# Strassen's scheme for two MLPs over pairs of batches, and attention in head pairs

## What is computed

```python
q_n, k_n = rmsnorm(q, g_q), rmsnorm(k, g_k)          # q, k, v: (4, 12, 448, 64)
attn = softmax(q_n @ k_n.T / 8);  x = attn @ v       # then x: (4, 448, 768)
xn = (x - mean) / sqrt(var + 1e-6) * g_ln            # first MLP
x = x + relu(xn @ w_ch1) @ w_ch2                     # 768 -> 3072 -> 768
u = x + (x.T @ U @ V).T                              # mixing over the 448 rows, rank 32
out = u + relu(u @ w2_ch1) @ w2_ch2                  # second MLP
```

## Time and profile before

| | us |
|---|---|
| runs before, median of 3 | 1796.21 (1795.0 to 1798.2) |
| profiled execution, span | 1794.6 |
| TensorE busy | 1766.4 |
| VectorE busy | 913.4 |
| ScalarE busy | 706.3 |
| GpSimd busy | 202.1 |

### The profile page before, as it was taken

The page is one execution under the profiler, slowest core; times in us unless marked ns, Lnnn a source line. Parts: engine busy times, 40 slices in busy tenths (PEclk is TensorE's granted clock), DMA queues, the critical chain, the costliest instruction groups (busy, mean ns, idle before and its releaser), DMA issues.

```text
span 1794.6 us, 29017 instructions
## 1 busy us (share of the span) xinstructions
PE 1766.4 (98%) x10272; PEld 1655.9 (92%) x10272; DVE 913.4 (51%) x1595; ACT 706.3 (39%) x1268; POOL 202.1 (11%) x201
## 2 busy tenths in 40 slices
PE   6999999999999999999999999999999999999998
PEld 5999999899999999999999999999999999999997
DVE  7999999743344444444444444444433433343332
ACT  5777777522333323332333233323222322232221
POOL 6666666000000000000000000000000000000000
PEclk9999999999999999999999999999999999999999
DMA  2222224233333233333333333332433333333320
GB/s 73 69 69 72 68 71 139 87 106 116 113 106 103 93 111 101 106 106 106 105 108 100 102 100 106 106 106 89 138 121 106 97 131 121 106 99 128 121 88 31
DMA packets 205744, 180.41 MB, mean 101 GB/s; under 512 B 12497, under 2 KB 179281, under 8 KB 205649
## 3 DMA queue, kind: packets, MB, share of 16 engines
q1 hardware_dynamic: 203280, 173.51, 30.3%
q10 hardware_dynamic: 2368, 5.51, 0.8%
HBM read 173.48 MB, written 5.51 MB: 100 GB/s over the span
## 4 chain that ended last, share of the span: by engine, by line
PE 80%; DVE 0%; issue 0%; ACT 0%
PE h_ps L733 39%; PE y_ps L750 38%; PE h_ps L680 1%; PE h_ps L669 1%; PE h_ps L698 1%; PE h_ps L706 0%; PE y_ps L658 0%; DVE in_nat L891 0%; ACT in_hi L786 0%; DVE in_lo L854 0%; DVE in_lo L851 0%; DVE y_t L927 0%
## 5 line engine op out<-in xcount | busy, mean ns | idle before, releaser
L844 DVE TENSOR_TENSOR w_lo<-w_raw,w_hi 128x768 fp32r<-128x768 f32 x190 | 182.0, 958 | 674.0 <-ACT w_hi L782 674.0
L750 PE MATMUL y_ps<-h_hi,w_hi 128*128 128x448 f32 x1152 | 424.4, 368 | 0.0
L733 PE MATMUL h_ps<-in_hi,w_hi 128*128 128x448 f32 x1152 | 415.9, 361 | 3.1 <-DVE in_lo L851 1.1
L733 PE MATMUL h_ps<-in_hi,w_lo 128*128 128x448 f32 x1152 | 417.9, 363 | 0.0
L750 PE MATMUL y_ps<-h_hi,w_lo 128*128 128x448 f32 x1152 | 417.8, 363 | 0.0
L750 PE MATMUL y_ps<-h_lo,w_hi 128*128 128x448 f32 x1152 | 417.7, 363 | 0.0
L733 PE MATMUL h_ps<-in_lo,w_hi 128*128 128x448 f32 x1152 | 417.4, 362 | 0.0
L781 ACT ACTIVATE w_hi<-w_raw 128x768 fp32r<-128x768 f32 x189 | 159.7, 845 | 538.1 <-PE y_ps L750 538.1
L817 ACT ACTIVATE h_hi<-h_ps 128x448 fp32r<-128x448 f32 x192 | 104.7, 545 | 380.1 <-PE h_ps L733 338.5
L733 PEld LDWEIGHTS h_ps<-in_hi,w_hi 128*128 128x128 f32 x1152 | 215.6, 187 | 19.1 <-DVE in_lo L851 1.5
L733 PEld LDWEIGHTS h_ps<-in_lo,w_hi 128*128 128x128 f32 x1152 | 216.2, 188 | 15.8
(11 more groups left out here) (90 smaller groups left out, 1407.3 us busy)
## 6 DMA issues: line engine op xcount, KB each, us to landing
w_raw<-in_moe_w_ch SPq DMA_DIRECT2D x384, 384.0 KB, 3.8
qk_raw<-in_q SPq DMA_DIRECT2D x48, 112.0 KB, 2.0
qk_raw<-in_k SPq DMA_DIRECT2D x48, 112.0 KB, 2.1
qt_raw<-in_q_t SPq DMA_DIRECT2D x48, 112.0 KB, 2.5
v_nat<-in_v SPq DMA_DIRECT2D x48, 112.0 KB, 2.0
out<-o_nat ACTq DMA_DIRECT2D x12, 336.0 KB, 5.0
out<-in_nat ACTq DMA_DIRECT2D x4, 336.0 KB, 3.1
u_sb<-in_moe_U SPq DMA_DIRECT2D x4, 56.0 KB, 2.5
```

Of the source, the lines that this page charges most:

```text
L733: last = nc.tensor.matmul(h_ps[j % 2][:, :S], w[:, j % NW, c, :], x[:, c, :], start=(c == 0 and t == 0), stop=(c == DC - 1 and t == 2))
L750: last = nc.tensor.matmul(y_ps[c][:, :S], w[:, j % NW, c * P:(c + 1) * P], x[:, j % 2, :], start=(j == 0 and t == 0), stop=(j == FC - 1 an ...
L844: nc.vector.tensor_tensor(w1_lo[:, r], w1_raw[:, r], w1_hi[:, r].bitcast(F32), ALU.subtract)
```

## The change

Both parts are written anew.

**MLPs.** Four units (`s` = 0 to 3) take two batches through one MLP each. Each product of 2x2 blocks is made with seven block products (P1 to P7) for eight, by Strassen's scheme in Winograd's form. The left factor is the weights, the right one the activations; both need sums of blocks first, and the seven products are combined after. An up-group ("G", 12 in a unit) has 3 blocks of depth, 9 matmuls a product; a down-group ("M", 18 in a unit) has 2 blocks of depth, 6 matmuls. The list `prods` sets one order for all engines: two up-groups, the first two products of the next, three down-groups. Six PSUM banks go round; P2, P3 and P4 are added onto the bank of P1, P5 and P7 after these were read (`ONTO`). The sums of weights (`weight_sum`) and of the hidden values (`hidden_sums`) are made on GpSimd, as are the low parts of P4's weights, the last of each group (`ON_POOL`); the other low parts (`weight_low`, L1063) on VectorE, 384 columns for G and 256 for M. `combine` and `gather` read the products on VectorE. The input of the next unit is split (`make_high`, `make_low`) beside the last 21 products. Results stand transposed in SBUF (`acc`) and go through DRAM (`xres`, `xnrm`) between units. The mixing has 12 items of two blocks, spread over the units 1 and 2.

**Attention.** 24 pairs of heads, 96 steps of 2 x 112 rows. The scores are six matmuls of 448 columns with 64 rows each (`score`, L705), head 0 in rows 0 to 63 and head 1 in 64 to 127. One maximum (L1003) covers both heads. The low part of q is made on GpSimd, and the power there is over 16 columns. x is turned back and normalised here (L736), not in the MLPs. Inputs arrive in other layouts, and the output leaves transposed.

```diff
+P1, P7, P6, P5, P2, P3, P4 = range(7)
+ORDER = {"G": (P1, P7, P6, P5, P2, P3, P4), "M": (P1, P5, P6, P2, P7, P3, P4)}
+ONTO = {P2: P1, P3: P5, P4: P7}
+LAST_IN_BANK = (P6, P2, P3, P4)
+HEAD = 2
+ON_POOL = {("G", P4), ("M", P4)}
...
+    for s in range(STAGES):
+        for j in range(NJ):
+            for g in (2 * j, 2 * j + 1):
+                prods += [("G", s, g, k) for k in ORDER["G"][HEAD if g == 2 * j and j else 0:]]
+            if j + 1 < NJ:
+                prods += [("G", s, 2 * j + 2, k) for k in ORDER["G"][:HEAD]]
+            prods += [("M", s, j * NM + m, k) for m in range(NM) for k in ORDER["M"]]
+    number = {p: q for q, p in enumerate(prods)}
...
+    for s in range(1, STAGES):
+        first = number["M", s - 1, NJ * NM - NM, P1]
+        anchors = (first + 3, first + 8, first + 12)
...
+                def squares(t):
...
+                    raw = qk[:, t % 2].rearrange("p a h i d -> p (a h i d)")
+                    nc.gpsimd.tensor_tensor(qk_sq[:].rearrange("p a h i d -> p (a h i d)"), raw, raw,
+                                            ALU.mult).then_inc(sq_done, 1)
...
+                def weight_sum(r, k):
...
+                    if k == P5:
+                        out, in0, in1, op = s1, a21, a22, ALU.add
+                    if k == P7:
+                        out, in0, in1, op = a21, a11, a21, ALU.subtract
...
+                    if k == P6:
+                        out, in0, in1, op = s2, s1, a11, ALU.subtract
...
+                    if k == P3:
+                        out, in0, in1, op = weights(product_of(r, P3)), a12, s2, ALU.subtract
...
+                    nc.gpsimd.tensor_tensor(out, in0, in1, op).then_inc(sum_done, 1)
+                def weight_low(q):
+                    pool.wait_ge(whi_done, q + 1)
+                    w = width(q)
+                    nc.gpsimd.tensor_tensor(w_lo[:, q % RING, :w], weights(q), w_hi[:, q % RING, :w].bitcast(F32),
+                                            ALU.subtract).then_inc(wplo_done, 1)
+                def hidden_sums(q):
+                    if (g := group_past(q, 1)) is not None:
+                        pool.wait_ge(relu_done, 4 * g + 3)
+                        if g:
+                            pool.wait_ge(hlo_done, cut(g - 1, P5))
+                        nc.gpsimd.tensor_tensor(t_t1, t_c12, t_b11, ALU.subtract).then_inc(th_done, 1)
+                        pool.wait_ge(th_done, 4 * g + 1)
+                        nc.gpsimd.tensor_tensor(t_c12, t_c22, t_t1, ALU.subtract).then_inc(th_done, 1)
+                        pool.wait_ge(th_done, 4 * g + 2)
+                        pool.wait_ge(hlo_done, cut(g, P1))
+                        nc.gpsimd.tensor_tensor(t_b11, t_c12, t_b11, ALU.subtract).then_inc(th_done, 1)
+                    if (g := group_past(q, 3)) is not None:
+                        pool.wait_ge(th_done, 4 * g + 3)
+                        pool.wait_ge(relu_done, 4 * g + 4)
+                        pool.wait_ge(hlo_done, cut(g, P2))
+                        nc.gpsimd.tensor_tensor(t_c21, t_c21, t_c12, ALU.subtract).then_inc(th_done, 1)
...
-                    lhs = q_st[:, slot, i * TP:(i + 1) * TP]
-                    nc.tensor.matmul(scores[i][:TP, :S], lhs, k_hi[:, slot, :], start=True, stop=False)
-                    nc.tensor.matmul(scores[i][:TP, :S], lhs, k_lo[:, slot, :], start=False,
-                                     stop=True).then_inc(scores_done, 1)
+                def score(n):
...
+                    for a, b in ((q_hi, k_hi), (q_hi, k_lo), (q_lo, k_hi)):
+                        for h in range(2):
+                            rows = slice(h * D, (h + 1) * D)
+                            last = nc.tensor.matmul(mm_ps[:TP, 2 * (n % 2) + h, :S], a[rows, t % 2, i * TP:(i + 1) * TP],
+                                                    b[rows, t % 2], start=a is q_hi and b is k_hi, stop=a is q_lo)
+                    last.then_inc(s_done, 1)
...
-                terms = ((w1_hi, in_hi), (w1_hi, in_lo), (w1_lo, in_hi))
...
-                    for t, (w, x) in enumerate(terms):
-                        last = nc.tensor.matmul(h_ps[j % 2][:, :S], w[:, j % NW, c, :], x[:, c, :],
-                                                start=(c == 0 and t == 0), stop=(c == DC - 1 and t == 2))
-                    for t, (w, x) in enumerate(terms):
-                        last = nc.tensor.matmul(y_ps[c][:, :S], w[:, j % NW, c * P:(c + 1) * P], x[:, j % 2, :],
-                                                start=(j == 0 and t == 0), stop=(j == FC - 1 and t == 2))
+                def product(q):
+                    kind, s, n, k = prods[q]
+                    weights_split(pe, q)
+                    if before[q] is not None:
+                        read_out(pe, before[q])
...
+                    for c in range(chunks):
+                        if kind == "G" and n == 0:
+                            pe.wait_ge(inlo_done[c], made(s, k))
+                        for p, (w, x) in enumerate(((w_hi, x_hi), (w_hi, x_lo), (w_lo, x_hi))):
+                            last = nc.tensor.matmul(bank(q), w[:, q % RING, c * P:(c + 1) * P], x[:, k, c],
+                                                    start=k not in ONTO and c == 0 and p == 0,
+                                                    stop=c == chunks - 1 and p == 2, skip_group_check=k in ONTO)
+                    last.then_inc(prod_done, 1)
...
+                    nc.vector.reduce_max(nmax[:, n % 2], mm_ps[:TP, 2 * (n % 2):2 * (n % 2) + 2, :S], axis=AX,
+                                         negate=True).then_inc(max_done, 1)
...
+                def weight_low(q):
+                    dve.wait_ge(whi_done, q + 1)
+                    w = width(q)
+                    nc.vector.tensor_tensor(w_lo[:, q % RING, :w], weights(q), w_hi[:, q % RING, :w].bitcast(F32),
+                                            ALU.subtract).then_inc(wlo_done, 1)
...
+                    nc.vector.tensor_tensor(in_lo[:, k, c], src, in_hi[:, k, c].bitcast(F32),
+                                            ALU.subtract).then_inc(inlo_done[c], 1)
+                    nc.vector.tensor_tensor(h_lo[:, k, g % 2], src, h_hi[:, k, g % 2].bitcast(F32), ALU.subtract
+                                            ).then_inc(hlo_done, 1)
+                def combine(q):
+                    g, k = g_no(q), prods[q][3]
...
+                    dve.wait_ge(prod_done, q + 1)
+                    if k == P6:
+                        dve.wait_ge(p1_done, g + 1)
+                        nc.vector.tensor_tensor(t_u2, bank(q), t_u2, ALU.add).then_inc(comb_done, 1)
+                        dve.wait_ge(comb_done, 5 * g + 1)
+                        wait(dve, th_done, 4 * g - 1)
+                        nc.vector.tensor_tensor(t_c22, bank(number[prods[q][:3] + (P7,)]), t_u2, ALU.add
+                                                ).then_inc(comb_done, 1)
+                        return
+                    if k == P5:
+                        dve.wait_ge(comb_done, 5 * g + 2)
+                        nc.vector.tensor_tensor(t_c22, bank(q), t_c22, ALU.add).then_inc(comb_done, 1)
+                    if k == P3:
+                        nc.vector.tensor_tensor(t_c12, bank(q), t_u2, ALU.add).then_inc(comb_done, 1)
+                    if k == P4:
+                        dve.wait_ge(comb_done, 5 * g + 4)
+                        nc.vector.tensor_tensor(t_c21, bank(q), t_u2, ALU.add).then_inc(comb_done, 1)
+                def gather(q):
+                    _, s, n, k = prods[q]
+                    j, m = divmod(n, NM)
+                    dve.wait_ge(prod_done, q + 1)
...
+                    to = {P1: u_acc[:, m], P6: u_acc[:, m], P7: acc[:, 1, m + HC], P5: acc[:, 1, m + HC],
+                          P2: acc[:, 0, m], P3: acc[:, 1, m], P4: acc[:, 0, m + HC]}[k]
...
+                    nc.vector.tensor_tensor(to, bank(q), to, ALU.add).then_inc(ev_done, 1)
```

1675 lines of the change are left out of this document (925 added, 750 removed).

## The result

The changed kernel takes **2004.11 us** (median of four runs, 1979.48 to 2041.47), the kernel before 1795.62: a ratio of 1.111, with a 95% interval of 1.1042 to 1.1177. The ratio and its interval leave out the run of 2041.47, which counts as a slow one, so they lie a little under the quotient of the two medians. It is slower by 11%, where 7% faster was forecast. The profiled execution took 1999.57 us, and its span is 1997.7.

The account below looks back on a forecast made before the run. TensorE was taken as the bound, with VectorE just hidden in the MLPs. Start 15, attention 350 + 8 + 6, products 1210, mixing 30, borders 25, lock 15, end 6: 1665 us of span, 1666 us measured; range 1600 to 1760.

Parts of the forecast that it names:

- +15 over the four units: MLPs: the part of VectorE's lock against GpSimd's SBUF reads expected to show in the time, 15 us.
- 0.12 us for each of 285 instructions: MLPs: mean lock wait of VectorE's two-SBUF-operand instructions, taking GpSimd's arrivals as random; 34 us a unit.
- 275 to 292 of 302 us: MLPs: VectorE's load per unit with the lock, against 302 us of TensorE products; just under the bound.
- Rival 2: MLPs: VectorE becomes the bound, 0.25 us lock for each of 285 instructions; +64, 1730 us; chance 0.15.
- rival 3: MLPs: the lock makes the kernel slower than before, from 0.36 us per instruction; 1900 us at 0.45; chance 0.08.
- the bank of P7: Down-products: P4 is added onto this bank after one product; VectorE lateness over 0.45 us stops TensorE there.
- the three borders: Between MLP units: VectorE's work in the last 21 products exceeds TensorE's 25.2 us; with accumulator loading, +25 us.
- The prediction's last sentence: Attention: if TensorE's pauses lower the clock's grant below 1.00, all attention terms are too low; no size given.
- Borders and mixing: MLPs: time beside the products; +25 us at unit borders, +30 for mixing items and turns of normalised x.
- 3.65 us a step: Attention: time of each of 96 steps, between 3.3 and 4.0; 350 us in all.
- rival 1: Attention: score matmuls of two heads take turns instead of running together; +24, 1690 us; chance 0.13.
- the two bounds: Attention: six score matmuls a step take 0.60 us if the heads run together, 1.20 if each takes 0.20.

Follow-up runs that it names:

- e1: Changed kernel with every GpSimd addition and subtraction for the MLPs replaced by a memset of the same tile, results left out; 1787.57 us.
- e4: Changed kernel with VectorE's weight and h splits in the first and last units reading one operand from PSUM, results left out; 1995.72 us.
- e13: Changed kernel with 168 VectorE weight splits around the turn from up- to down-products cut to 16 columns; 1928.02 us, MLPs 1482.6.
- e14: Changed kernel with 179 VectorE weight splits in the middle of the down-products cut to 16 columns; 1982.27 us, MLPs 1542.8.
- e16: e11 with the makings of the first unit's input 9 instead of 8 steps apart, nothing left out; 1933.46 us, median of four.
- e11: Changed kernel, attention only: maximum in PSUM, root of the variance earlier on GpSimd, two wide matmuls in each of the first 8 steps; 1951.59 us.
- e3: Changed kernel with the low parts of P4's weights made on VectorE instead of GpSimd; 2031.0 us, MLPs 1546.9.
- e5: Changed kernel with the six score matmuls of a step on all 128 rows, scores of single heads left out; 1993.12 us.
- e6: Changed kernel with two more matmuls of 128 rows and 448 columns ahead of every step's scores, nothing left out; 2079.93 us.

## Why the prediction was wrong

**The step that failed: "I put what shows of it at +15 over the four units".** Two things are wrong in it. The size is the smaller one: 0.12 us for each of 285 instructions came from half of 0.55 times GpSimd's share of the time. Measured are 0.27 in the mean, and 0.38 for the splits of h (999 less 620 ns). The engines do not meet at random; the sums of h on GpSimd and the splits of h on VectorE belong to the same turn, and both engines' instructions grow while they meet. VectorE's own work was reckoned well: without the lock it is 249 us a unit (994.3 over four, e1), for 228 and the mixing's 17 in two units. The larger error is the way from load to time. The prediction added VectorE's work over a whole unit, found 275 to 292 of 302 us, and let it hide. VectorE was in fact busy 331 of 400. Yet TensorE lost time, since in the 24 us around each turn VectorE had no gap at all. The kernel whose GpSimd reads nothing puts the price at 195 us (1549.8 less 1354.8), 13 times the term; e4, with 36.5 of 42.0 us in the fourth unit, says that nearly all of it is the lock. e13 against e14 shows the place: 67 us from 86 us of work taken away there, 7 from 55 elsewhere.

**Rivals 2 and 3** named the mechanism and their tests read it right: a mean of over 0.98 us for 448 columns was to be rival 3, and 0.999 came. But they too turned it into time over the unit. Rival 2's 0.25 us for each instruction should have given 1730 us, and the measured 0.27 gave 2004. Rival 3 set its threshold at 0.36 and its place at the bank of P7. The waits for `acc` and `u_acc`, for the readings of all banks together, are about 36 us in all, against 83.2 for `h_lo`. The place was the turn; the prediction did add up a burst, but only at the three borders.

**What of the 195 us is the clock.** In the changed kernel a tenth of the MLPs' time (clock 0.95) runs at 1.2 GHz, 151 us, with the memsets about a fiftieth, 31 us. As an estimate, these 120 us more at half pace are worth up to 60 us. The prediction's last sentence named such a loss for attention alone and gave it no price and no chance.

**The MLPs apart from the lock: 1355 for 1265.** Matmuls that follow one another without a pause start 0.203 us apart in some stretches of e1 (54 steps from 1600.20 to 1611.14) and 0.207 in others (50 steps from 1705.66 to 1715.99), both down-products, where the earlier trace rows had 0.200. In the mean over e1 it is 0.2035: 6048 of them are 1231 us, +21. Why they are further apart was not tried. The last unit, with neither mixing nor a next input, takes 319.5 us in e1, 12 more than its share of these: +47 for four, of which the 31 us at half pace can be some 15. Borders and mixing make the other three units longer by 77 together, for 55 forecast: +22.

**Attention: the step right, the clock not.** 3.65 us a step and 96 x 3.65 = 350 us were forecast. At full clock the maxima of the changed kernel come mostly 3.2 to 3.9 us apart, and in e16, from the first at 17.5 to the last at 366.7, 95 steps take 349.2 us: 3.68 each. The score matmuls of two heads start together, so rival 1 falls. The three pairs start at 189.12, 189.42 and 189.62 and the values at 189.92: the scores take 0.80 us a step, neither the 0.60 nor the 1.20 of the two bounds, so that 3.65 came out right as a value between them, not because a term was known. The Trainium skill ("TensorE: Matmul & The Clock Gate", "Part 3: Packing small matmuls — row/col tiling") says that matmuls in distinct row groups run concurrently. The trace agrees for these 64 rows, though not with the 0.60 that was worked out from it. The first score came at 14.8 us for 15. What was missing are 71 us (424.5 less 353.5): slow steps at the start until the clock rose (at 53 us), and three stretches at 1.2 GHz. Ahead of the first and the third of these the small product of VectorE took 1.83 and 1.47 us, and the third falls within ScalarE's wait for one load. GpSimd's in-order queue, which e11 changed too, was not tried alone. The prediction had the makings of the first input as 21 splits of 0.54 on VectorE, +8; their load, their sums on GpSimd and their place in ScalarE's queue were not counted.

**The named part of the change**, low parts on GpSimd, was costed among GpSimd's 167 us as covered. e3 confirms that it hardly matters to either side: 1546.9 against 1549.8, less than unchanged MLPs differ.

**The lock rule.** The Trainium skill ("SBUF — State Buffer", "Who interferes with whom") says that a VectorE instruction with two SBUF inputs contends with a GpSimd instruction that reads SBUF. The runs here agree: 999 ns for 448 columns with both operands in SBUF, 620 when GpSimd only writes; and with one operand in PSUM 84 of them are busy 50.4 us instead of 81.8.

## What to carry to other kernels

Price a lock or an engine's load where the bursts are, by adding up all that stands on the engine between two points that TensorE must pass, never over the mean of a stage. An engine at 83% can be the bound. Before sums are moved to GpSimd, ask which two-operand SBUF instructions VectorE has at the same time, and whether one of the operands can lie in PSUM. And ask of each pause of TensorE what the clock does after it: here a pause of 1 to 4 us was followed by up to 61 us at half pace, and filler matmuls that left the cause in place made it worse.

## What the runs showed that was not expected

- A fall of the clock lasts much longer in attention than in the MLPs. With the narrow matmuls of attention the stretches at half clock lasted mostly 10 to 65 us, with TensorE busy 96 to 100% of the time; with the 128 rows and 448 columns of the MLPs 3 to 10 us. In e5, whose scores take all 128 rows, those of attention lasted 3 to 7 us; in e6, with two wide matmuls beside the narrow ones, 7 to 51. That the kind of matmul is the reason fits this, but was not tried by itself.
- At the start the clock column says 1.00 while TensorE works at half pace (203 instructions in 40 us for 367). How long differs from run to run of the same attention, from 28 to 205 us. That may be most of the spread of 1979 to 2041 us; only one of those four runs has a profile. Wide matmuls in the first steps ended it at 19 to 22 us in all five kernels that had them.
- A copy on GpSimd that reads one SBUF operand lengthens VectorE's splits of 448 columns too, from 0.62 to 0.73 us; a memset does not at all (0.62).
- GpSimd loses too: its sums of h (448 columns) take 1.27 to 1.43 us in the mean, and its work in the fourth unit fell from 209.0 to 182.3 us when VectorE read PSUM.
- The lock may reach further than two-operand instructions. VectorE's normalisation of 128 columns (L1057, one tensor and two numbers a row, all in SBUF) takes 0.31 us at the least and 1.28 at the most. No run tried it by itself.
